# Window attention on Trainium2: keys of v in blocks of 128 on all partitions, put together on chip

## The reference

```python
mask_plain = (rel >= 0) & (rel < window)                                  # window = 32
mask_dil = (rel >= 0) & (rel < window * dilation) & (rel % dilation == 0) # dilation = 4
attn = softmax(where(mask, q @ k.T / 8, -1e9)); out = attn @ v
```

## Time and profile before

| | |
|---|---|
| runs, median (lowest to highest) | 757.04 us (757.02 to 757.27), 3 runs |
| the profiled execution, its own time | 761.43 us |
| its span, first to last instruction | 759.6 us |
| granted TensorE clock, mean of the span | 0.954 of 2.4 GHz |
| busy: TensorE, VectorE, GpSimd, ScalarE | 688.5, 434.0, 335.6, 316.7 us |
| attention stage: first matmul, last matmul of `values` | 6.36 us to 94.15 us |
| DMA, mean over the span | 126 GB/s |
| DMA, mean over the first 100 us | 238 GB/s |

### The profile page before, as it was taken

One profiled execution on the slowest core, in us unless ns is written; L12 is line 12 of the kernel. 1 busy time (PEld: TensorE's weight loads), 2 busy tenths in 40 slices (PEclk: granted clock), 3 DMA queues, 4 the chain that ended last, 5 costly groups with the idle time before them and its releaser, 6 DMA issues.

```text
span 759.6 us, 13697 instructions
## 1 busy us (share of the span) xinstructions
PE 688.5 (91%) x4720; PEld 611.7 (81%) x4721; DVE 434.0 (57%) x951; ACT 316.7 (42%) x579; POOL 335.6 (44%) x333
## 2 busy tenths in 40 slices
PE   4779985399999996879999999999999999999997
PEld 3557752399999995769898998999899989999996
DVE  4446756465435556565555669555556785665552
ACT  3657842233312343343334354534333554343433
POOL 1232100353223234183545697545548965654621
PEclk9978998599999999789999999999999999999999
DMA  8996679259436760601201114310101123011102
GB/s 238 286 330 174 200 258 379 79 204 338 176 146 225 274 254 26 213 28 29 56 28 56 34 51 139 111 56 28 56 29 56 45 67 111 28 57 56 28 1 84
DMA packets 44998, 95.61 MB, mean 126 GB/s; under 512 B 6644, under 2 KB 17908, under 8 KB 43792
## 3 DMA queue, kind: packets, MB, share of 16 engines
q1 hardware_dynamic: 42944, 91.00, 36.1%
q0 software_dynamic: 2000, 3.91, 1.4%
HBM read 85.22 MB, written 12.32 MB: 128 GB/s over the span
## 4 chain that ended last, share of the span: by engine, by line
PE 73%; DVE 10%; DMA 6%; issue 5%; POOL 2%; SPq 2%; ACT 1%; DVEq 0%; POOLq 0%; ACTq 0%
PE H_ps L1358 10%; PE prod L1394 9%; PE prod L1389 9%; PE prod L1390 9%; PE out_ps L1417 6%; PE out_ps L1418 6%; PE out_ps L1416 6%; DMA x_rows<-xo 3%; PE Y_ps L1369 2%; PE Y_ps L1371 2%; PE Y_ps L1370 2%; PE O_ps L1271 2%; DVE xs_lo L1129 2%; PE T_ps L1260 2%; PE S_ps L1252 2%
## 5 line engine op out<-in xcount | busy, mean ns | idle before, releaser
L1389 PE MATMUL prod<-xs_hi,ab_hi 128*128 128x384 f32 x490 | 167.4, 342 | 5.6 <-DVE sig L1218 2.4
L1390 PE MATMUL prod<-xs_hi,ab_lo 128*128 128x384 f32 x490 | 166.3, 339 | 0.0
L1394 PE MATMUL prod<-xs_lo,ab_hi 128*128 128x384 f32 x490 | 126.9, 340 | 2.8 <-DVE xs_lo L1129 2.8
L1389 PEld LDWEIGHTS prod<-xs_hi,ab_hi 128*128 128x128 f32 x490 | 92.6, 189 | 18.2 <-DVE sig L1218 4.4
L1390 PEld LDWEIGHTS prod<-xs_hi,ab_lo 128*128 128x128 f32 x490 | 92.4, 189 | 9.0
L1394 PEld LDWEIGHTS prod<-xs_lo,ab_hi 128*128 128x128 f32 x490 | 89.5, 189 | 3.7 <-DVE xs_lo L1129 3.7
L1418 PE MATMUL out_ps<-o_hi,h_lo 128*128 128x512 f32 x216 | 85.8, 397 | 0.0
L1417 PE MATMUL out_ps<-o_lo,h_hi 128*128 128x512 f32 x216 | 85.7, 397 | 0.0
L1416 PE MATMUL out_ps<-o_hi,h_hi 128*128 128x512 f32 x216 | 85.6, 396 | 0.0
L1358 PEld LDWEIGHTS H_ps<-xgT,w_sb 128*128 128x128 f32 x704 | 82.3, 196 | 2.4 <-DVE xgT L1068 1.6
L1358 PE MATMUL H_ps<-xgT,w_sb 128*128 128x128 f32 x704 | 82.5, 279 | 1.2 <-DVE xgT L1068 1.2
(11 more groups left out here) (193 smaller groups left out, 1328.5 us busy)
## 6 DMA issues: line engine op xcount, KB each, us to landing
w_sb<-w_dram SPq DMA_DIRECT2D x32, 512.0 KB, 5.7
w_raw<-w_dram SPq DMA_DIRECT2D x32, 512.0 KB, 6.1
ab<-gv_dram SPq DMA_DIRECT2D x36, 384.0 KB, 3.1
v_raw<-v_dram SPq DMA_DIRECT2D x3, 1728.0 KB, 12.2
ab<-gv_dram SPq DMA_DIRECT2D x36, 128.0 KB, 3.1
xb<-x_rows SPq DMA_DIRECT2D x18, 256.0 KB, 4.3
out_dram<-o_sb SPq DMA_DIRECT2D x18, 256.0 KB, 2.0
x_rows<-xo SPq DMA_DIRECT2D x60, 64.0 KB, 4.9
```

Of the source, the lines that this page charges most:

```text
L1389: mm(dst[:, 0:HB], ab_hi[at][:, w, c], xs_hi[:, x - 1, c], start=(c == 0), stop=False)
L1390: mm(dst[:, 0:HB], ab_lo[at][:, w, c], xs_hi[:, x - 1, c], start=False, stop=False)
L1394: last = mm(dst[:, 0:HB], ab_hi[at][:, w, c], xs_lo[:, x - 1, c], start=False, stop=(c == 1))
```

## The change

- The host lays v out with 32 positions of zeros ahead of the 576 and 32 behind, and cuts these 640 into 5 blocks of 128 keys (`blocks`): 128 partitions, 1280 KB for a batch. `v_raw` is [128, 5, 512] with a buffer for each batch, and the wait ahead of batch 3's load is gone.
- k gets 32 positions of zeros ahead of its 576, and the 32 positions where its two parts meet are stored in both: 224 and 416 positions for a head, 1280 KB for a batch instead of 1152. Tile 0 now takes its 96 keys from the padding on, with a mask that leaves the padding out.
- q and k of each batch are stored in DRAM and in SBUF as "first positions of all heads, then the rest of all heads" (`columns` with split), so that the first pieces are contiguous: for each partition 3072 bytes of q and 3584 of k in place of 4 runs of 768 bytes. v's first piece is 2 blocks.
- An even tile's 96 keys lie in one block, on partitions 0 to 95. An odd tile's first 64 keys lie on partitions 64 to 127 of one block and its last 32 on partitions 0 to 31 of the next. GpSimd copies them to the same partitions of `v_one` with two chained copies; rows 32 to 63 of the odd tiles of `v_one` are set to zero once. TensorE transposes an odd tile's exponentials with two matmuls against `ident` for each pair of heads, 64 columns of weights into PSUM partitions 64 to 127 and 32 columns into 0 to 31, so 8 in place of 4; `values` and the copy to `pT_sb` take 128 rows in odd steps. 4 of a batch's 9 tiles are odd, 16 of the 36.
- VectorE clears both `T_ps` at the start, and GpSimd sets the ones of `v_one`.
- The routing weights come from the host as one array [128, 36], in one transfer after step 17.
- `XO_SLOTS` is 9, and the loads of batches 2 and 3 are issued after steps 1, 3, 5 and 10, 12, 14.

The diff, cut to its core (`take_v` is a chained `g.tensor_copy` of the rows given, and `at_query` and `at_key` give the slices of a tile in the new layout):

```diff
-XO_SLOTS = 6
-V_SLOTS = 3
-LOADS = {0: (2, "q"), 2: (2, "k"), 4: (2, "v"), 7: (3, "q"), 9: (3, "k"), 11: (3, "v")}
+XO_SLOTS = 9
+FIRST_Q, FIRST_K, FIRST_V = FIRST_TILES * QT, FIRST_TILES * QT + WINDOW, 2
+KEYS = SEQ + 2 * WINDOW
+LOADS = {1: (2, "q"), 3: (2, "k"), 5: (2, "v"), 10: (3, "q"), 12: (3, "k"), 14: (3, "v")}
+ROUTE_W = 17
...
-                sp.dma_start(q_sb[0][:, :, cols], qT[0].rearrange("p (h s) -> p h s", h=HPK)[:, :, cols]).then_inc(qk_sem, 16)
-                sp.dma_start(k_sb[0][:, :, cols], kT[0].rearrange("p (h s) -> p h s", h=HPK)[:, :, cols]).then_inc(qk_sem, 16)
-                sp.dma_start(v_raw[0][:, tiles], v_tiles[0, :, tiles]).then_inc(v_sem, 16)
+            sp.dma_start(q_sb[0][:, 0:first_q], qT[0, :, 0:first_q]).then_inc(first_qk_in, 16)
+            sp.dma_start(k_sb[0][:, 0:first_k], kT[0, :, 0:first_k]).then_inc(first_qk_in, 16)
+            sp.dma_start(v_first[:, 0:first_v], v[0, :, 0:first_v]).then_inc(first_v_in, 16)
...
-            sp.dma_start(w_route[:, :, 0:E], w_gate.rearrange("(c p) e -> p c e", p=P),
-                         allow_slow_non_contiguous=True).then_inc(route_w_in, 16)
-            sp.dma_start(w_route[:, :, E:E + 1], w_skip.rearrange("(c p e) -> p c e", p=P, e=1),
-                         allow_slow_non_contiguous=True).then_inc(route_w_in, 16)
...
+                if s == ROUTE_W:
+                    sp.dma_start(w_route[:].rearrange("p c e -> p (c e)"), w_r).then_inc(route_w_in, 16)
...
-                g.tensor_copy(v_one[:, t, :, 0:HD], v_raw[b % V_SLOTS][:, t].rearrange("p (h d) -> p h d", h=HEADS))\
-                    .then_inc(v_ready, 1)
+                if t % 2 == 0:
+                    take_v(b, t, slice(0, KT), t // 2)
+                else:
+                    take_v(b, t, slice(QT, P), t // 2)
+                    take_v(b, t, slice(0, WINDOW), t // 2 + 1)
+                pool.sem_inc(v_ready)
...
-            a.activation(pT_sb[:, s % 2], T_ps[s % 2][0:KT], ACT.Copy).then_inc(pT_copied, 1)
+            rows = slice(0, KT if ORDER[s][1] % 2 == 0 else P)
+            a.activation(pT_sb[rows, s % 2], T_ps[s % 2][rows], ACT.Copy).then_inc(pT_copied, 1)
...
-            v_.memset(v_one[:, :, :, HD:HD + 1], 1.0).then_inc(ones_set, 1)
+            for i in range(2):
+                v_.memset(T_ps[i][:], 0.0).then_inc(weights_cleared, 1)
...
-                    i = nc.tensor.transpose(T_ps[s % 2][0:KT, n], p_sb[:, s % 3, n], ident[:])
+                    if ORDER[s][1] % 2 == 0:
+                        i = nc.tensor.transpose(T_ps[s % 2][0:KT, n], p_sb[:, s % 3, n], ident[:])
+                    else:
+                        mm(T_ps[s % 2][QT:P, n], p_sb[:, s % 3, n, 0:QT], ident[:], start=True, stop=True)
+                        i = mm(T_ps[s % 2][0:WINDOW, n], p_sb[:, s % 3, n, QT:KT], ident[:], start=True, stop=True)
...
-                        i = mm(O_ps[s % 2][own, n, 0:HD + 1], pT_sb[:, s % 2, n, own], v_one[:, t, kind * HPK + n], start=True, stop=True)
+                        keys = slice(0, KT if t % 2 == 0 else P)
+                        i = mm(O_ps[s % 2][own, n, 0:HD + 1], pT_sb[keys, s % 2, n, own], v_one[keys, t, kind * HPK + n],
+                               start=True, stop=True)
```

More of the change, by code:

```diff
@@ L144, in build_program @@
         with ExitStack() as att:
[L146 to L149, removed]
+            q_sb = [sb(att, f"q_sb{i}", [P, HPK * SEQ]) for i in range(BATCH)]
+            k_sb = [sb(att, f"k_sb{i}", [P, HPK * KEYS]) for i in range(BATCH)]
+            v_raw = [sb(att, f"v_raw{i}", [P, V_BLOCKS, HEADS * HD]) for i in range(BATCH)]
+            v_one = sb(att, "v_one", [P, NT, HEADS, HD + 1])
             p_sb = sb(att, "p_sb", [P, 3, HPK, KT])
-            pT_sb = sb(att, "pT_sb", [KT, 2, HPK, P])
+            pT_sb = sb(att, "pT_sb", [P, 2, HPK, P])
             xo = sb(att, "xo", [P, XO_SLOTS, HPK, HD])
@@ L286, in build_program @@
         ones_set = sem("ones_set")
+        weights_cleared = sem("weights_cleared")
+        v_taken = sem("v_taken")
         v_ready = sem("v_ready")
@@ L590, in _, with take_v @@
             assert chain.n == IDENT_STEPS
+            g.memset(v_one[:, :, :, HD:HD + 1], 1.0).then_inc(ones_set, 1)
             pool.wait_ge(ones_set, 1)
+            g.memset(v_one[WINDOW:QT, 1:NT:2], 0.0).then_inc(ones_set, 1)
+            pool.wait_ge(ones_set, 2)
+            chain = Chain(pool, v_taken)
+            def take_v(b, t, rows, n):
+                chain(g.tensor_copy(v_one[rows, t, :, 0:HD], v_raw[b][rows, n].rearrange("p (h d) -> p h d", h=HEADS)))
             for s, (b, t) in enumerate(ORDER):
@@ L934, in _ @@
             chain(v_.tensor_scalar(ahead[:], cols_f[:], query[:, 0:1], None, ALU.subtract))
[L935 to L939 removed]
+            v_.tensor_scalar(no_key[:], cols_f[:], float(WINDOW), MASKED, ALU.is_lt, ALU.mult)
+            v_.tensor_scalar(too_early[:], ahead[:], 1.0, MASKED, ALU.is_lt, ALU.mult)
+            chain(v_.tensor_scalar(too_late[:], ahead[:], float(WINDOW), MASKED, ALU.is_gt, ALU.mult))
+            chain(v_.tensor_tensor(masks[:, 1], too_early[:], too_late[:], ALU.add))
+            v_.tensor_tensor(masks[:, 0], masks[:, 1], no_key[:], ALU.add)
             for n, at in enumerate(CUTS):
@@ L1251, in scores @@
                             rows, h = slice(HD * row, HD * row + HD), kind * PAIRED + slot
-                            i = mm(S_ps[s % 2][row][QT * kind:QT * kind + QT, slot, 0:KT], q_sb[b][rows, h, QT * t:QT * t + QT],
-                                   k_sb[b][rows, h, key_start(t):key_start(t) + KT], start=True, stop=True)
+                            i = mm(S_ps[s % 2][row][QT * kind:QT * kind + QT, slot, 0:KT], q_sb[b][rows, at_query(t, h)], k_sb[b][rows, at_key(t, h)], start=True, stop=True)
                 i.then_inc(scores_ready, 1)
@@ L1508, in by_kind, with columns, blocks, routing @@
         return np.stack([x[:, 0], dilated], axis=1)
-    def columns(x):
-        x = by_kind(x).reshape(BATCH, KINDS, 2, PAIRED, SEQ, HD)
-        return np.ascontiguousarray(x.transpose(0, 2, 5, 1, 3, 4)).reshape(BATCH, P, HPK * SEQ)
-    def windows(x):
-        x = by_kind(x).transpose(0, 3, 1, 2, 4)
-        starts = [0] + [QT * t - WINDOW for t in range(1, NT)]
-        x = np.stack([x[:, s:s + KT] for s in starts], axis=2)
-        return np.ascontiguousarray(x).reshape(BATCH, KT, NT * HEADS * HD)
+    def columns(x, pad, split, again):
+        x = by_kind(x).reshape(BATCH, KINDS, 2, PAIRED, SEQ, HD).transpose(0, 2, 5, 1, 3, 4).reshape(BATCH, P, HPK, SEQ)
+        x = np.pad(x, ((0, 0), (0, 0), (0, 0), (pad, 0)))
+        return np.concatenate([x[..., 0:split].reshape(BATCH, P, -1), x[..., split - again:].reshape(BATCH, P, -1)], axis=2)
+    def blocks(x):
+        x = np.pad(by_kind(x).transpose(0, 3, 1, 2, 4), ((0, 0), (WINDOW, WINDOW), (0, 0), (0, 0), (0, 0)))
+        return x.reshape(BATCH, V_BLOCKS, P, HEADS * HD).transpose(0, 2, 1, 3).reshape(BATCH, P, V_BLOCKS * HEADS * HD)
+    def routing(gate, skip):
+        both = np.concatenate([np.asarray(gate), np.asarray(skip).reshape(D, 1)], axis=1)
+        return both.reshape(DC, P, E + 1).transpose(1, 0, 2).reshape(P, DC * (E + 1))
     def by_feature(gate, value):
@@ L1527 @@
     arrays = {
-        "qT": columns(q), "kT": columns(k),
-        "v": windows(v),
-        "w_skip": moe_w_skip, "w_gate": moe_w_gate, "w1": moe_w1, "w2": moe_w2,
+        "qT": columns(q, 0, FIRST_Q, 0), "kT": columns(k, WINDOW, FIRST_K, WINDOW),
+        "v": blocks(v),
+        "w_r": routing(moe_w_gate, moe_w_skip), "w1": moe_w1, "w2": moe_w2,
         "gv": by_feature(np.asarray(moe2_w_gate), np.asarray(moe2_w_val)),
```

47 lines of the change are left out of this document (28 added, 19 removed).

## The result

The changed kernel takes 774.37 us (median of 4, 771.26 to 778.74) against 757.03 us of the kernel before beside it (756.05 to 757.27): a ratio of 1.0236, 95% interval 1.0185 to 1.0286. It is **slower by 17 us**, where 12 us faster was forecast, and lies beyond the range. So the two traces differ by 9.8 us only, and the parts have to be compared by their places in the traces, not by the spans.

A forecast was written before the change was run, and what follows sets the result against it. Attention was taken as half bound by transfers, half by TensorE. From the median 757.04, 20.3 us saved on transfers and 7.9 added on TensorE gave 744.6 us, range 735.5 to 761 (742 to 748 without rivals).

The forecast's parts named there:

- The bound before: Attention stage: one half bound by transfers, one by TensorE; 18.1 us were waits for DMA and the lower clock.
- the transfers: Attention's loads and stores: all 18.1 us of waits go and step 3 starts earlier, ending values at 73.85, 20.3 us earlier.
- Step 3: Attention step waiting for the rest of q and k: start at 12.5 us, 2.2 earlier, ends 11.5 and 13.3.
- What is added on TensorE: Odd attention steps: 8 matmuls stand for 4 transposes, adding 7.9 us in all, without cover.
- one after the other without a gap, 4 x 0.11 = 0.44: Odd steps' matmuls: extra us per step at full clock, 0.88 in steps 1 and 3; chance 0.38.
- The upper bound of 1.35: Odd steps' matmuls: extra us per step if each of the eight pays the 0.13 drain, 8 x 0.24 - 0.57.
- The row taken as the nearest: Trace rows where weights of 128 columns and of 9 alternate; read as showing no gap, supporting 0.44 us.
- A drain at each change: Rival, odd steps: the array's division changes eight times, 22.7 us added, 759.4 us for the kernel; chance 0.35.
- Side by side: Rival, odd steps: a pair's two matmuls overlap, so nothing is added on TensorE, 736.7 us; chance 0.17.
- The queue stays the bound: Rival, transfers: v's blocks move little faster or small stores hold the queue, 754.5 us at 247 GB/s; chance 0.10.
- What was called hidden: GpSimd's added copies, VectorE's clearing of two banks and SyncE's read of rows, all expected to cost 0.
- The cover, step 3's wait for its load: Attention's start: waiting until 12.5 us covers step 0's maxima coming up to 2.3 us later through VectorE's clearing.

The follow-up runs named there:

- e5: Changed kernel with GpSimd's copies putting odd tiles' keys together, so every tile is transposed whole and nothing is cleared: 743.27 us, ratio 0.980.
- e6: e5 with the routing stage's rows read earlier, at steps 20, 22, 24 and 30 instead of 24, 26, 28 and 33: 739.25 us, ratio 0.9736.
- e9: e5 with 6 slots of xo instead of 9: 744.38 us, ratio 0.9818.
- e12: e6 with VectorE's split of the routing weights moved from behind its last step to behind steps 30 and 31: 739.40 us, ratio 0.9757.
- e8: e5 with v in windows of 96 keys on 96 partitions and three buffers, as before the change: 751.26 us, ratio 0.9898.
- e10: e8 with each v window 128 keys long on 128 partitions, the last 32 never used: 742.91 us, ratio 0.9771.
- e13: Kernel before with only v's windows made 128 keys long on 128 partitions, the last 32 never used: 753.41 us, ratio 0.990.
- e7: e5 with the routing weights loaded as before the change, two transfers of tiny pieces behind batch 1's v: 745.19 us, ratio 0.9835.
- e1: Kernel before with odd tiles' four transposes written as four plain matmuls by the identity, same 96 columns: 757.51 us, ratio 0.9997.
- e2: Changed kernel with an odd step's four 64-column matmuls first, then the four 32-column ones, 2 division changes instead of 8: 759.98 us, ratio 1.0021.
- e11: Changed kernel run again without an edit: 774.02 us, ratio 1.0209.
- e3: Changed kernel with the 32-column piece widened to 64 and p_sb's unused columns cleared instead of T_ps: 745.53 us, ratio 0.9828.

## Why the prediction was wrong

- **The bound before, and the transfers: right.** Step 3 came at 12.02 (12.5), waits for stores and for later k vanished, DMA ran at 426 GB/s. With TensorE's work left as it was, the attention ended at 75.59 and 76.61 us (e5, e6) against 73.85: step 3 started 0.8 and 0.4 us earlier than forecast, steps 3 to 5 took 8.7 and 8.8 us instead of 7.75, nearly all of it at the lower speed, and stops at two later steps cost 1.7 and 1.9. The same loads ended it at 73.13 and 74.23 in e9 and e12. For the whole kernel, e5's ratio is 757 x 0.020 = 15.1 us where the forecast has 20.3, because of the wait for rows; e6, with the rows read earlier, which the change doesn't do, has 757 x 0.0264 = 20.0. The largest part that a run separates is v's partitions (e8 against e10: 11.9 us of the attention; e13: 7.9 alone on the kernel before). The forecast put part of v's gain down to fewer bytes and some 2 us to the routing weights' pieces; e10 and e7 show neither. Step 0 came 1.1 us earlier than the forecast had it (5.25 against 6.36), which gained nothing.
- **What is added on TensorE: wrong, and this is the step that failed.** The term "one after the other without a gap, 4 x 0.11 = 0.44" measured 2.22 us a step. Two things were missed. The 0.11 us is a transpose's; a plain float32 matmul of 128 columns is two such passes, 0.22 (e1). And the drain of 0.13, which I had as a rival at 0.35, comes at each change between 64 and 32 columns (e2). Together 8 x (0.22 + 0.13) = 2.8 us, the burst measured 2.79. The upper bound of 1.35 carried the first fault too, and so the range ended at 761 instead of near 773: with 16 x 2.22 the sum is 757.04 - 20.3 + 35.5 = 772.2, measured 774.4. That it comes so near is partly luck: by these terms the attention ends 15.2 us later than before, and it ended 13.1 later in the first trace, where TensorE was fast from 15 us on, and 17.4 later in e11.
- The first fault could have been read from the rows: `scores` and `values` are 8 matmuls each in the code and "x16" in the earlier trace rows, the four transposes "x4". (The 16 matmuls given for each of them in the section on the kernel before are records, not instructions.)
- **The row taken as the nearest was not near.** 128 columns and 9 of the earlier trace rows follow each other without a gap, but neither is a division into 64 or 32. The nearer row was the 0.13 between bursts in the earlier trace rows. The Trainium skill's rule (TensorEngine Tiling (Array Packing), Key Properties), that changing the tiling mode drains TensorE, holds for 128x64 and 128x32 here: 0.13 us each time.
- **A drain at each change** (rival): its mechanism is one half of what happened, and its price of 1.35 us lacks the other half, the second pass. **Side by side** (rival): right as a mechanism, for pieces of one width (e3), which these are not. **The queue stays the bound** (rival): not here.
- **What was called hidden: nearly right.** GpSimd's copies stayed at 0.607 us and in TensorE's shadow. VectorE's clearing took 1.02 us for both banks, and the first maxima came 1.5 us later than the earlier trace rows; TensorE's wait of 3.0 us for `row_min` is its mark. The cover, step 3's wait for its load, fell short: in e5, which clears nothing, the load was there at 11.66, and here step 3 follows the work before it without idle time at 12.02. So the forecast's 12.5 was nearly met, but it was VectorE and not the load that set the start. The read of rows was free only while the attention was long (e5). The masks took longer as well, with GpSimd's copies running beside them: 1.79 us against 1.38 before in the first trace, and 2.76 in e11 (third line below), whose step 3 started at 13.00. That the copies are the cause wasn't tested.

```profile
7.12 1.79 DVE L985 SCALAR_TENSOR_TENSOR masks<-before,begun,masks 128x96 bf16<-128x96 f32 x4
8.95 0.26 DVE L990 CUSTOM_DVE_ANT_0 p_sb<-S_ps,masks 128x96 f32<-128x96 f32 x1
...
7.12 2.76 DVE L985 SCALAR_TENSOR_TENSOR masks<-before,begun,masks 128x96 bf16<-128x96 f32 x4
```

- **Behind the attention** the shift of 13.1 us shrank to 11.8 at the routing stage's first matmul (108.50 against 96.68), as the wait for the routing weights' split was 1.3 us shorter there. At the end of the routing stage some 11 us are left, and they stay nearly whole to the end of the kernel: 10.1 between the spans. The medians differ by 17.3; the other 7.2 us are the 4.4 by which the profiled execution of before lay above its median and some 3 by which that of after lay below.

## What to carry to other kernels

Count an instruction in the trace before you price it: if the code's 8 matmuls are 16 records and its 4 transposes are 4, a transpose's duration is half a matmul's, and replacing one by the other doubles it. Pieces of one width can run side by side, pieces of two widths pay a drain at every turn, so a useless half can be the cheapest thing in the kernel. And look at what partitions a load covers before its bytes: padding 96 partitions to 128 moved a third more data in less time, and a copy that GpSimd makes anyway can do the shifting that TensorE was asked for.

## What the runs showed of the hardware

- A plain float32 matmul of 128 columns by weights of 128 rows takes two records of 0.109 us start to start, a transpose of the same one.
- Changing between weights of 64 and of 32 columns costs 0.13 us at each change (e2: 6 fewer, 0.78 us less). Changing only between partitions 0 to 63 and 64 to 127 of the result, at 64 columns, costs nothing; the pieces start together (e3: 0.92 us for 16 records).
- A copy on GpSimd of 512 columns takes 0.61 us on 96, 64 or 32 partitions, moved to other partitions or not.
- Packets of 18432 bytes took 1.26 and 1.28 us in the median where the transfer covers partitions 0 to 95 (e8, kernel before) and 0.69 where it covers all 128 (e10, e13).
- The same kernel can run its matmuls at the low speed until 23 us (e11) or reach the high one near 15 (first trace). The granted clock is given as 1.00 either way, as the clock records begin only there; before that the length of a matmul tells the speed.
